# Attention in front of two mixture-of-experts layers: the score rows of a tile as three blocks of 384 keys instead of 512 + 512 + 128

## What is computed

```python
def _attn_ref(q, k, v):                       # (4, 8, 1152, 64) each, fp32
    q_pool = q.reshape(B, H, S // 2, 2, D).mean(axis=3)      # 576 pooled queries
    scores = scale * np.matmul(q_pool, k.transpose(0, 1, 3, 2))   # 576 x 1152
    scores = scores - np.max(scores, axis=-1, keepdims=True)
    attn = np.exp(scores)
    attn = attn / (np.sum(attn, axis=-1, keepdims=True) + 1e-09)
    return np.matmul(attn, v)

x = attention, laid out as 2304 rows of 512
x = eight experts, one chosen per row (512 -> 1024 -> 512), scaled by two gates
x = silu(x @ w_gate) * (x @ w_val) @ w_out          # 512 -> 1536 -> 512
```

## Time and profile before

| | us |
|---|---|
| median of 3 runs | 1480.16 |
| lowest and highest | 1476.31, 1483.12 |
| the profiled execution | 1476.28 |
| its span in the trace | 1474.5 |
| attention in the span | about 24 to 608 |

### The profile page before, as it was taken

How to read it: one execution, slowest core, us unless ns; L and a number is a source line. 1 busy time by engine, 2 the same in 40 slices (tenths; PEclk the granted TensorE clock), 3 DMA queues, 4 the chain that set the end, 5 groups by cost and what they waited for, 6 DMA issues and landing times. The chain is left out here.

```text
span 1474.5 us, 24891 instructions
## 1 busy us (share of the span) xinstructions
PE 1377.8 (93%) x7733; PEld 1195.3 (81%) x7734; DVE 873.2 (59%) x1658; ACT 638.4 (43%) x1549; POOL 345.2 (23%) x241
## 2 busy tenths in 40 slices
PE   3999999999999999739978999998999999999998
PEld 2788888888888888537767787887999999999997
DVE  2899999999999998673443444445632323223232
ACT  2888888788888887532034102004411111111111
POOL 3122222222222220279179205022101010100000
PEclk9999999999999999969998999999999999999999
DMA  7566666666666764356256313114400000000000
GB/s 164 124 139 139 138 138 142 146 144 145 145 149 145 195 132 153 101 193 247 88 199 233 116 43 107 43 57 142 150 32 15 29 15 17 26 0 21 0 22 22
DMA packets 127931, 156.85 MB, mean 106 GB/s; under 512 B 47633, under 2 KB 86545, under 8 KB 125841
## 3 DMA queue, kind: packets, MB, share of 16 engines
q1 hardware_dynamic: 111968, 114.35, 30.8%
q10 hardware_dynamic: 12880, 31.99, 6.5%
q0 software_dynamic: 3040, 9.96, 2.0%
HBM read 87.33 MB, written 29.10 MB: 79 GB/s over the span
## 5 line engine op out<-in xcount | busy, mean ns | idle before, releaser
L514 ACT ACTIVATE p_hi<-ps_t 128x512 fp32r<-128x512 f32 (+1 forms) x336 | 194.3, 586 | 69.1 <-PE ps_t L694 64.7
L657 DVE TENSOR_TENSOR p_lo<-ps_t,p_hi 128x512 fp32r<-128x512 f32 (+1 forms) x336 | 216.9, 666 | 12.4 <-ACT p_hi L514 7.8
L578 DVE TENSOR_REDUCE maxima<-ps_s 128x1 f32<-128x512 f32 x288 | 193.7, 686 | 41.5 <-PE ps_s L792 37.7
L538 ACT ACTIVATE probs<-ps_s,neg_max 128x512 f32<-128x512 f32 x288 | 198.6, 690 | 44.1 <-DVE neg_max L591 43.9
L792 PE MATMUL ps_s<-kq_t 128*128 128x512 f32 x640 | 199.7, 414 | 13.6 <-DMA kq_t<-kept_rows 9.5
L694 PE MATMUL ps_t<-ident,probs 128*128 128x128 f32 x1296 | 198.5, 274 | 1.4 <-DVE kept_rows L569 0.8
L1026 POOL TENSOR_TENSOR w_parts<-raw_w,w_parts 128x1024 fp32r<-128x1024 f32 x64 | 150.9, 2396 | 184.5 <-ACT w_parts L1096 184.4
L694 PEld LDWEIGHTS ps_t<-ident,probs 128*128 128x128 f32 x1296 | 156.0, 140 | 46.3 <-DVE p_lo L657 9.6
L1642 ACT ACTIVATE silu<-ps_g 128x384 f32<-128x384 f32 x72 | 35.4, 491 | 314.6 <-PE ps_g L1748 314.6
L1695 DVE TENSOR_TENSOR silu<-ps_g,silu 128x384 f32<-128x384 f32 x72 | 40.1, 558 | 210.7 <-ACT silu L1642 210.7
L1096 ACT ACTIVATE w_parts<-raw_w 128x1024 fp32r<-128x1024 f32 x64 | 67.1, 1059 | 220.0 <-PE ps_h L1423 104.2
(11 more groups left out here) (190 smaller groups left out, 2786.5 us busy)
## 6 DMA issues: line engine op xcount, KB each, us to landing
raw_w<-in_moe_w ACTq DMA_DIRECT2D x61, 512.0 KB, 4.1
kq_t<-kept_rows SPq DMA_DIRECT2D x32, 608.0 KB, 6.2
kq_t<-kept_rows SPq DMA_DIRECT2D x32, 320.0 KB, 7.1
raw_k<-in_k SPq DMA_DIRECT2D x32, 288.0 KB, 5.7
raw_v<-in_v SPq DMA_DIRECT2D x16, 576.0 KB, 5.5
kq_t<-kept_rows SPq DMA_DIRECT2D x32, 288.0 KB, 6.5
raw_q<-in_q SPq DMA_DIRECT2D x32, 256.0 KB, 4.1
y_by_slot<-x_out SPq DMA_DIRECT2D x25, 256.0 KB, 2.0
```

The lines of the kernel that those rows point to most:

```text
L514: nc.scalar.activation(p_hi[prob_ring(kind, m)][:, 0:w], T[ring(kind, j)][:, 0:w], ACT.Copy).then_inc(hi_ready, 1)
L538: nc.scalar.activation(probs[:, at:at + 512], S[(2 * tile + h) % SR][:, :], ACT.Exp, bias=neg_max[:, tile:tile + 1], accum_out=sums[par][: ...
L578: nc.vector.reduce_max(maxima[:, 3 * tile + h:3 * tile + h + 1], S[(2 * tile + h) % SR][:, :], AX).then_inc(max_done, 1)
L657: nc.vector.tensor_tensor(p_lo[n][:, 0:w], t[:, 0:w], p_hi[n][:, 0:w].bitcast(F32), ALU.subtract).then_inc(t_free, 1)
```

## The change

The score row of a tile is made in three blocks of 384 keys (`BLK`), each in a bank alone. The bank `R`, `scores_rem`, `exp_rem`, `largest_rest` and their two semaphores are gone. The blocks use four banks: blocks 1 and 2 of every tile always banks 1 and 2, block 0 in turn banks 0 and 3 (`bank`). Every block has its own maximum and its own exponential. The exponentials of a tile run in the order block 1, block 2, block 0. The steps c, g, x of a pair and all three tables of places are set anew. The other two layers are untouched.

```diff
-    MAIN = 8 * P
+    BLK = SK // 3
...
     UNITS = [
         ("b", 0), ("b", 1), ("b", 2), ("b", 3), ("b", 4), ("b", 5), ("b", 6), ("b", 7), ("b", 8),
-        ("g", 0), ("g", 1), ("c", 0), ("c", 1), ("c", 2), ("g", 2), ("a", 0), ("g", 3), ("a", 1),
-        ("a", 2), ("x", 0), ("a", 3), ("x", 1), ("a", 4), ("a", 5), ("a", 6), ("a", 7), ("a", 8),
+        ("g", 0), ("c", 0), ("c", 1), ("g", 1), ("c", 2), ("g", 2), ("g", 3), ("a", 0), ("a", 1),
+        ("x", 0), ("a", 2), ("x", 1), ("a", 3), ("a", 4), ("a", 5), ("a", 6), ("a", 7), ("a", 8),
     ]
-    SCORES_AT = [(26, 26), (2, 2), (4, 5), (7, 8), (12, 13), (17, 17), (19, 20), (21, 22), (23, 24)]
-    MAXIMA_AT = [(25, 25), (2, 2), (3, 4), (7, 8), (12, 13), (16, 16), (18, 19), (20, 21), (22, 23)]
-    EXP_AT = [(0, 2, 2), (4, 4, 4), (7, 8, 8), (11, 11, 13), (16, 16, 17), (18, 19, 20), (21, 21, 21), (22, 23, 23), (25, 25, 25)]
+    SCORES_AT = [(25, 26, 26), (2, 2, 2), (4, 5, 5), (6, 7, 7), (8, 12, 12), (12, 14, 15), (18, 18, 19), (20, 21, 22), (23, 24, 24)]
+    MAXIMA_AT = [(25, 25, 25), (2, 2, 2), (4, 4, 4), (6, 6, 6), (7, 11, 11), (11, 13, 15), (17, 18, 18), (19, 20, 21), (22, 23, 23)]
+    EXP_ORDER = (1, 2, 0)
+    EXP_AT = [(0, 2, 2), (4, 4, 4), (6, 6, 7), (8, 9, 11), (13, 13, 15), (16, 17, 19), (19, 20, 21), (23, 23, 24), (25, 25, 25)]
...
-        S = [ps(f"ps_s{i}", 512) for i in range(SR)]
-        R = ps("ps_r", 512)
+        S = [ps(f"ps_s{i}", 512) for i in range(4)]
...
+        def bank(par, tile, b):
+            return S[b if b else 3 * ((par + tile) % 2)][:, 0:BLK]
...
+                def exps(p, par, kind, tile, b):
+                    if b == EXP_ORDER[0]:
                         act.wait_ge(bias_ready, TILES * p + tile + 1)
...
+                    at = tile * SK + b * BLK
+                    nc.scalar.activation(probs[:, at:at + BLK], bank(par, tile, b), ACT.Exp,
                                          bias=neg_max[:, tile:tile + 1],
+                                         accum_out=sums[par][:, sum_col(tile, b)]).then_inc(exp_done, 1)
...
+                def largest(p, par, tile, b):
+                    dve.wait_ge(s_ready, 3 * (TILES * p + tile) + b + 1)
+                    nc.vector.reduce_max(maxima[:, 3 * tile + b:3 * tile + b + 1], bank(par, tile, b), AX
+                                         ).then_inc(max_done, 1)
+                    if b == 2:
+                        dve.wait_ge(max_done, 3 * (TILES * p + tile + 1))
+                        nc.vector.tensor_reduce(neg_max[:, tile:tile + 1], maxima[:, 3 * tile:3 * tile + 3], AX,
+                                                ALU.max, negate=True).then_inc(bias_ready, 1)
...
+                def scores(p, par, tile, b, opening=False):
+                    if not (opening and (tile == 0 or (tile == 1 and b == 0))):
+                        pe.wait_ge(exp_done, 3 * (TILES * p + tile - 1) + b)
...
                     for n, (w, head) in enumerate(ops):
+                        at = head * HEAD + b * BLK
+                        last = nc.tensor.matmul(bank(par, tile, b), w, kq_t[par][:, at:at + BLK],
                                                 start=(n == 0), stop=(n == len(ops) - 1))
                     last.then_inc(s_ready, 1)
```

More of the change, by code:

```diff
@@ L104, in attention @@
     TR = 3
-    SR = 3
     LAST = PAIRS - 1
@@ L112, in attention @@
         ("b", 0), ("b", 1), ("b", 2), ("b", 3), ("b", 4), ("b", 5), ("b", 6), ("b", 7), ("b", 8),
[2 rows of a table removed]
-    ]
-    SCORES_AT = [(26, 26), (2, 2), (4, 5), (7, 8), (12, 13), (17, 17), (19, 20), (21, 22), (23, 24)]
-    MAXIMA_AT = [(25, 25), (2, 2), (3, 4), (7, 8), (12, 13), (16, 16), (18, 19), (20, 21), (22, 23)]
-    EXP_AT = [(0, 2, 2), (4, 4, 4), (7, 8, 8), (11, 11, 13), (16, 16, 17), (18, 19, 20), (21, 21, 21), (22, 23, 23), (25, 25, 25)]
[2 rows of a table added]
+    ]
+    SCORES_AT = [(25, 26, 26), (2, 2, 2), (4, 5, 5), (6, 7, 7), (8, 12, 12), (12, 14, 15), (18, 18, 19), (20, 21, 22), (23, 24, 24)]
+    MAXIMA_AT = [(25, 25, 25), (2, 2, 2), (4, 4, 4), (6, 6, 6), (7, 11, 11), (11, 13, 15), (17, 18, 18), (19, 20, 21), (22, 23, 23)]
+    EXP_ORDER = (1, 2, 0)
+    EXP_AT = [(0, 2, 2), (4, 4, 4), (6, 6, 7), (8, 9, 11), (13, 13, 15), (16, 17, 19), (19, 20, 21), (23, 23, 24), (25, 25, 25)]
     assert X_LOADS[X_EARLY - 1][1] * P <= (B - 1) * SQ and (B - 1) * HP <= LAST - 1
     assert w1.shape[2] == PIECE
-    assert HALF_SCALE == 0.25 and len(UNITS) % TR == 0 and 2 * TILES % SR == 0
+    assert HALF_SCALE == 0.25 and len(UNITS) % TR == 0 and 3 * BLK == SK and BLK <= 512
     KEEP = {"first": "ag", "mid": "abcxg", "last": "abcx", "tail": "bcx"}
@@ L222, in attention @@
         s_ready = sem("s_ready")
-        r_ready = sem("r_ready")
         max_done = sem("max_done")
         bias_ready = sem("bias_ready")
-        exp_rem_done = sem("exp_rem_done")
         exp_done = sem("exp_done")
@@ L536, in exp_half @@
                             act.wait_ge(t_filled, upto(p, kind, every, UNIT_LAST["c"]))
-                    at = tile * SK + h * 512
-                    nc.scalar.activation(probs[:, at:at + 512], S[(2 * tile + h) % SR][:, :], ACT.Exp,
+                    at = tile * SK + b * BLK
+                    nc.scalar.activation(probs[:, at:at + BLK], bank(par, tile, b), ACT.Exp,
                                          bias=neg_max[:, tile:tile + 1],
-                                         accum_out=sums[par][:, sum_col(tile, h)]).then_inc(exp_done, 1)
+                                         accum_out=sums[par][:, sum_col(tile, b)]).then_inc(exp_done, 1)
                 def body(p, par, kind):
@@ L548, in body @@
                         for tile in range(TILES):
[L549 to L554, removed]
+                            for at, b in zip(EXP_AT[tile], EXP_ORDER):
+                                if kind != "tail" and at == n:
+                                    exps(p, par, kind, tile, b)
                 for g in range(GROUPS):
@@ L618, in normalisers @@
                 def normalisers(p, par):
-                    dve.wait_ge(exp_done, 2 * TILES * p)
+                    dve.wait_ge(exp_done, 3 * TILES * p)
                     s3 = sums[1 - par][:, :].rearrange("p (t s) -> p t s", s=3)
@@ L670, in body @@
                                 continue
[L671 to L676, removed]
+                            of = (p, par) if tile else (p + 1, 1 - par)
+                            for b in range(3):
+                                if MAXIMA_AT[tile][b] == n:
+                                    largest(*of, tile, b)
                     if kind == "tail":
@@ L684, in _ @@
                     group_lo(g, g % TR)
-                largest_half(0, 0, 0)
-                largest_half(0, 0, 1)
-                largest_rest(0, 0)
+                for b in range(3):
+                    largest(0, 0, 0, b)
                 over_pairs(dve, body)
@@ L708, in fill @@
                     if what in "ab":
-                        done = 2 * TILES * p + (2 * QT if what == "a" else -2)
+                        done = 3 * (TILES * p + (QT if what == "a" else -1))
                         pe.wait_ge(exp_done, done)
@@ L715, in fill @@
                     elif what == "c":
-                        pe.wait_ge(exp_done, 2 * TILES * p)
+                        pe.wait_ge(exp_done, 3 * TILES * p)
                         last = transposes(t, [probs[:, TC * SK + (3 * i + n) * P:TC * SK + (3 * i + n + 1) * P]
@@ L779, in operands @@
                             for h in heads for part in range(2)]
[L781 to L786, removed]
+                def scores(p, par, tile, b, opening=False):
+                    if not (opening and (tile == 0 or (tile == 1 and b == 0))):
+                        pe.wait_ge(exp_done, 3 * (TILES * p + tile - 1) + b)
+                    if tile in (0, QT) and b == 0:
                         pe.wait_ge(kq_copied[tile // QT], 16 * COPIES * (p + 1))
@@ L790, in scores @@
                     for n, (w, head) in enumerate(ops):
-                        at = head * HEAD + h * 512
-                        last = nc.tensor.matmul(S[(2 * tile + h) % SR][:, :], w, kq_t[par][:, at:at + 512],
+                        at = head * HEAD + b * BLK
+                        last = nc.tensor.matmul(bank(par, tile, b), w, kq_t[par][:, at:at + BLK],
                                                 start=(n == 0), stop=(n == len(ops) - 1))
                     last.then_inc(s_ready, 1)
[L796 to L807, removed]
                 def body(p, par, kind):
@@ L822, in body @@
                             opening = kind == "first" and tile > 0
[L823 to L828, removed]
+                            for b in range(3):
+                                if SCORES_AT[tile][b] == n:
+                                    scores(*of, tile, b, opening)
                     if kind == "tail":
@@ L841, in _ @@
                     group(g, T[g % TR]).then_inc(t_filled, 1)
```

(5 more changed lines are left out.)

## The result

| | before | after |
|---|---|---|
| median, us | 1479.99 (4 runs) | 1528.4 (4 runs) |
| lowest and highest | 1476.31, 1483.12 | 1524.79, 1529.7 |
| ratio | | 1.0324 [1.0294, 1.0354] |
| span of the profiled execution | 1474.5 | 1523.0 |

The forecast was 1462 us and faster. The page after shows the same number of instructions on PE and 96 more on DVE. Two of its lines look strange. PE's granted clock, which was 9 in every slice of the attention before, is 8 in several of the first 16. And the queue q14, whose kind is "instruction", so a queue that loads code, carries 48 packets (before: 18, with 0.14 MB). The lines are the busy times, PE's busy tenths and its clock in 40 slices, and the queue.

The account below looks back on a forecast made before the run. PE was taken as the bound, DVE close behind; 1.0 us less PE work and 0.1 less waiting cut the 35.16 us pair to 34.1, −16 us over 15 periods; with 2 us added toward the median, 1462 us, range 1449 to 1482.

Parts of the forecast that it names:

- Maxima on DVE: DVE's maxima per attention pair: 13.3 us before, 13.8 after; taken as 0.4 us more work, DVE 32.6 to 33.0.
- What is late next: Walk through the new order: PE work 32.95 us, DVE 33.0, waits 1.1 against 1.2, so the period becomes 34.1 us.
- C: Rival: maxima placed ahead of their scores make DVE wait 2.3 us a pair instead of 1.33; 1500 us, chance 0.09.
- The sign I had to watch for: Forecast fails if DVE stands still over 2 us a pair, with `maxima` waiting for `ps_s` leading its waits.
- Scores on PE: Score matmuls per pair: 60 of 384 columns at 0.173 us replace 40 of 512 and 20 of 128; saves 1.0 us.
- The other price weighed there: A 384-column score matmul on PE at 0.190 us, saving nothing; as a rival 1478 us, chance 0.04.
- The period: Attention time per pair, from the once-a-pair reciprocal: 35.16 us falls to 34.1; over 15 periods, −16 us.
- Products of c0: PE at step 13 waits for the copy of b8's result, DVE being 1.4 us late: wait 0.4 us.
- Products of a0: PE at step 19 waits for DVE's scaled copy of unit c: wait 0.4 us.
- Tile 7's block 1: The one place found where a score block waits for the exponential that frees its bank: 0.2 us.
- Products of b0: PE at step 3 waits for the copy of a8's result: the 0.5 us wait becomes 0.1.
- Moved steps: g3 and next tile 0 move a step earlier; cover between first head's key copies and tile 0 shrinks 4.6 to 3.5 us.

Follow-up runs that it names:

- a_pad30: The kernel after with 30 one-column memsets at the start of DVE's program, shifting its loop's code by 30 instructions: 1471.09 us against 1483.32 for the kernel before, ratio 0.9929.
- a_hint: The kernel after with a prefetch hint for DVE's jump back, one more instruction a turn: 1469.98 us, ratio 0.9909 to the kernel before.
- places 234: The kernel after with only the first instruction of DVE's loop moved, to place 234 of a 256-instruction code block: 1505.19 us, one run.
- the kernel before with fillers: The kernel before with 17 one-column memsets a pair (DVE's loop 283 instructions), its first instruction at place 239 of a code block: 1519.67 us; at place 0, 1491.79 us.
- a_slot239: The kernel after with only the first instruction of DVE's loop moved, to place 239 of a 256-instruction code block: 1505.38 us, one run.
- Place 215: The kernel after with only the first instruction of DVE's loop moved, to place 215 of a 256-instruction code block: 1472.01 us, one run.

## Why the prediction was wrong, step by step

- **The step that failed is the sum itself: it has no term for code.** "Maxima on DVE" counts the 0.4 us that 27 maxima a pair take beyond the 21 of before, and not that they make DVE's loop 33 instructions longer. "What is late next" then takes DVE's program as a list of durations. The runs put 57.9 us in that place. No rival held it: C has DVE stand still at scores not yet made, and those waits are 4 us in 400 once the stop is gone, against 15.1 before. The sign I had to watch for (DVE idle over 2 us a pair) did come, under another name: "issue". Without the stop the same kernel takes 1470 to 1471 us (`a_pad30`, `a_hint`), 8 us above the forecast: the rest of the sum had the direction right and about half of the gain per pair.
- **Scores on PE: right in size.** Eight matmuls of blocks in a clean pair take 247.95 − 246.56 = 1.39, 0.174 each; forecast 0.173. The other price weighed there, the one that saves nothing, is not seen.

```profile
246.56 1.56 PE L773 MATMUL ps_s<-kq_t 128*128 128x384 f32 x8
247.95 0.60 PE L674 MATMUL ps_t<-ident,probs 128*128 128x128 f32 x4
248.31 0.48 PE L741 MATMUL ps_o<-p_hi,v_hl 128*128 128x512 f32 x1
```

- **DVE's work: right.** 33.07 us in the clean window, forecast 33.0. **ACT: right**, 28.53 against 28.64 before.
- **The period: start and gain mis-sized.** My 35.16 was a mean with the last two pairs in it, which have less to do (33.95 and 32.23 before as after). The loop's own period was 35.47, and the last two have not become shorter. So the gain is to be taken over 13 pairs, and it is 0.59, not 1.06: 7.7 us of the 16.
- **The waits: the places right, the sizes mostly not, and one place missed.** In a clean pair on PE:

```profile
232.35 0.49 PE L674 MATMUL ps_t<-ident,probs 128*128 128x128 f32 x3
232.91 0.39 PE L750 MATMUL ps_o<-v_hl,p_hi 128*128 128x256 f32 x1
...
238.98 0.60 PE L674 MATMUL ps_t<-ident,probs 128*128 128x128 f32 x4
239.54 0.47 PE L741 MATMUL ps_o<-p_hi,v_hl 128*128 128x512 f32 x1
...
242.15 0.60 PE L674 MATMUL ps_t<-ident,probs 128*128 128x128 f32 x4
242.79 0.62 PE L773 MATMUL ps_s<-kq_t 128*128 128x384 f32 x2
243.25 0.60 PE L674 MATMUL ps_t<-ident,probs 128*128 128x128 f32 x4
...
253.60 0.87 PE L773 MATMUL ps_s<-kq_t 128*128 128x384 f32 x4
254.63 0.62 PE L773 MATMUL ps_s<-kq_t 128*128 128x384 f32 x2 [0.15 <-ACT probs L532]
255.09 0.60 PE L674 MATMUL ps_t<-ident,probs 128*128 128x128 f32 x4
```

  Products of c0: 0.56 instead of 0.24, +0.32 (forecast 0.4). Products of a0: 0.56 instead of 0.36, +0.20 (0.4). Tile 7's block 1: 0.64 and 0.46 instead of 0.36 and 0.35, +0.39 (0.2). Products of b0: no wait (0.1). Not foreseen: tile 1's last block, which must wait for an exponential of tile 0. The six matmuls of the tile take 1.49 instead of 1.04, +0.45. Together 1.36 against 1.1. Of the missing 0.47 us a pair (1.06 − 0.59) these places explain 0.26 more than forecast; the other 0.2 is not assigned.
- **Moved steps: right.** From 150 to 550 us PE waits for no copy of keys in `a_pad30`; the cover held.

## What to carry to other kernels

Count the instructions of each engine's loop, semaphore and register steps included, before adding any. Twelve short maxima cost 9.7 us a turn here, since with them the body reached a third code block, and a body just over one code block is free or dear by its place alone. In a profile the sign is an idle stretch whose releaser is "issue" at the same place in every turn, with a transfer of the code queue inside it. A remedy that adds an instruction also moves the code, so look at the code queue before you credit it. And a mean period over all pairs hides both the short last ones and an alternation of good and bad turns: list the single ones first.

## What the runs showed of the chip

- A jump back to a head that is no longer held stops DVE for 3.6 to 4.7 us (places 234 and 239, and the kernel before with fillers). In the kernel after the stop is 8.2 to 8.4 us, in two parts: 4.6 to 4.9 from the jump to the head, 4.1 from the head to the instruction behind it. ACT's loop of 278 instructions shows no such stop in either kernel; at which place it begins isn't known.
- The stop costs twice. PE stood still for 6.1 us at full clock, and its granted clock was then 0.50 for 6.8 to 10.2 us, most of it while PE had work again. After the shorter stops at place 239 (`a_slot239`) it was 3.4 us.
- Starting the loop on the first place of a code block cured the stops and cost 7 us once, in the opening. Place 215 cost less there (first reciprocal at 74.2 us, against 72.7 with the plain shift).
